# Attention with decay and two expert layers: the state added in PSUM, shared low parts moved to the first expert, alpha loaded ahead, zero matmuls out

## The reference

```python
for t in range(S):                      # attention: B=4, H=8, S=768, D=48
    state = alpha[:, :, t, :, None] * state + einsum('bhd,bhe->bhde', k[:, :, t], v[:, :, t])
    y[:, :, t] = einsum('bhd,bhde->bhe', q[:, :, t], state)
x = y as [3072, 384]
logits = x @ w_gate                     # greedy routing: 8 experts, 384 tokens each
h = relu(x[mask] @ w1[e]);  x[mask] = h @ w2[e]
g = x @ gate2                           # shared by all tokens
out = (g * sigmoid(g) * (x @ val2)) @ out2
```

## Time and profile before

| what | value |
|---|---|
| median of 3 runs | 927.67 us (926.37 to 929.67) |
| the profiled execution | 926.6 us |
| its span | 924.8 us |
| TensorE busy over the span | 854.6 us (92%) |
| VectorE | 528.2 us (57%) |
| ScalarE | 281.0 us (30%) |
| GpSimd | 233.5 us (25%) |
| mean granted TensorE clock | 0.959 of full |

### The profile page before, as it was taken

One profiled execution on the slowest core, in us unless ns is written; L12 is line 12 of the kernel. 1 busy time (PEld: TensorE's weight loads), 2 busy tenths in 40 slices (PEclk: granted clock), 3 DMA queues, 4 the chain that ended last, 5 costly groups with the idle time before them and its releaser, 6 DMA issues.

```text
span 924.8 us, 17511 instructions
## 1 busy us (share of the span) xinstructions
PE 854.6 (92%) x6606; PEld 800.6 (87%) x6606; DVE 528.2 (57%) x1098; ACT 281.0 (30%) x505; POOL 233.5 (25%) x171
## 2 busy tenths in 40 slices
PE   6899998249999999999999999999999999999991
PEld 3778776139999999999999999999999999999990
DVE  7999996654654465446445644563466446543330
ACT  1333333032234323432242224333233332333220
POOL 2433223013051314312340324041405030522001
PEclk7999999559999999999999999999999999999996
DMA  9688863040230023002200320041003002300000
GB/s 342 229 300 302 295 254 111 4 160 1 69 95 23 3 68 94 26 0 85 77 26 0 102 60 26 0 123 44 20 29 116 34 9 68 94 26 1 1 1 29
DMA packets 25570, 77.27 MB, mean 84 GB/s; under 512 B 3776, under 2 KB 10432, under 8 KB 22464
## 3 DMA queue, kind: packets, MB, share of 16 engines
q1 hardware_dynamic: 22464, 67.39, 21.2%
q0 software_dynamic: 3072, 9.44, 3.1%
HBM read 67.38 MB, written 9.44 MB: 83 GB/s over the span
## 4 chain that ended last, share of the span: by engine, by line
PE 76%; DVE 2%; issue 1%; DMA 1%; POOL 0%; ACT 0%; POOLq 0%; ACTq 0%
PE ps_up L1490 45%; PE ps_acc L1490 27%; PE ps_turn L774 2%; DMA x_tok<-x_rows,from_rows 1%; PE ps_turn L794 1%; PE ps_turn L1496 0%; DVE quick_marks_space L699 0%; PE ps_turn L779 0%; DVE quick_marks_space L751 0%; POOL out L1338 0%; PE ps_up L1496 0%; PE ps_acc L1496 0%; POOL x_tok L1310 0%; DVE quick_cut L698 0%; DVE quick_base L693 0%
## 5 line engine op out<-in xcount | busy, mean ns | idle before, releaser
L1316 POOL TENSOR_TENSOR w_low<-w_raw,w_high 128x768 fp32r<-128x768 f32 x60 | 134.8, 2254 | 293.7 <-ACT w_high L1380 293.4
L1490 PE MATMUL ps_up<-z_high,gated_high 128*128 128x384 f32 x576 | 198.1, 344 | 0.2 <-DVE z_low L1447 0.2
L1490 PE MATMUL ps_up<-z_high,gated_low 128*128 128x384 f32 x576 | 193.6, 336 | 0.0
L1490 PE MATMUL ps_up<-z_low,gated_high 128*128 128x384 f32 x576 | 193.4, 336 | 0.0
L1490 PEld LDWEIGHTS ps_up<-z_high,gated_high 128*128 128x128 f32 x576 | 108.2, 188 | 0.9 <-ACT z_high L1393 0.5
L1490 PEld LDWEIGHTS ps_up<-z_high,gated_low 128*128 128x128 f32 x576 | 108.3, 188 | 0.0
L1490 PEld LDWEIGHTS ps_up<-z_low,gated_high 128*128 128x128 f32 x576 | 108.1, 188 | 0.0
L1452 DVE TENSOR_TENSOR act_out<-ps_up,act_out 128x384 f32<-128x384 f32 x96 | 53.6, 558 | 94.4 <-ACT act_out L1396 86.0
L1399 ACT CAST u_high<-act_out 128x384 fp32r<-128x384 f32 x96 | 49.4, 514 | 160.4 <-DVE act_out L1456 160.4
L1490 PE MATMUL ps_acc<-gated_high,u_high 128*128 128x384 f32 x288 | 97.6, 339 | 0.3 <-DVE u_low L1459 0.3
L1490 PE MATMUL ps_acc<-gated_low,u_high 128*128 128x384 f32 x288 | 97.2, 337 | 0.0
(11 more groups left out here) (164 smaller groups left out, 1439.0 us busy)
## 6 DMA issues: line engine op xcount, KB each, us to landing
qka_in<-in_qka SPq DMA_DIRECT2D x24, 1026.0 KB, 7.5
w_raw<-in_experts SPq DMA_DIRECT2D x64, 384.0 KB, 3.1
v_in<-in_v SPq DMA_DIRECT2D x24, 192.0 KB, 7.4
x_rows<-y_rows SPq DMA_DIRECT2D x24, 192.0 KB, 3.6
quick_marks_space<-in_gated SPq DMA_DIRECT2D x6, 576.0 KB, 5.1
gated_raw<-in_gated SPq DMA_DIRECT2D x6, 576.0 KB, 6.1
x_tok<-x_rows,from_rows POOLq DMA_INDIRECT x24
out<-o_tok,to_rows POOLq DMA_INDIRECT x24
```

Source lines behind the costliest of these rows:

```text
L1316: pool.tensor_tensor(w.low[:, m % RING, :], w.raw[:, m % RING, :], w.high[:, m % RING, :].bitcast(F32), ALU.subtract).then_inc(w_low_ready, 1)
L1490: mm = pe.matmul(acc, lhs[a], rhs[b], start=(first and i == 0), stop=(last and i == 2))
```

## The change

It does five things.

1. The state is added in PSUM: for chunks after the first, `update` starts with one matmul of the identity with the state (128 x 192), and the key-value products accumulate on it. `advance` is one instruction that reads PSUM.
2. The two zero matmuls in front of each unit's scores go (the 22 warm-up matmuls at the start stay).
3. All 12 raw chunks of the shared weights have a place of their own during the attention. Only the high parts are cast there.
4. The 12 low parts are made in place by GpSimd in the first expert, between `split_rest(0)` and the splits for expert 1. TensorE waits for each in `gate_and_value`.
5. The first unit's load is cut in three (alpha, reverse alpha, queries and keys), each with a semaphore. The second unit's load comes next, before the identity, the turner, the mask and the first values.

```diff
-            for b in range(B):
-                if b < BUFFERS:
-                    load(b)
+            for cols, landed in ((slice(ALPHA_AT, BACK_AT), alpha0_in), (slice(BACK_AT, QKA), back0_in),
+                                 (slice(0, ALPHA_AT), qk0_in)):
+                sp.dma_start(qka_in[0][:, cols], qka[0, :, cols]).then_inc(landed, 16)
+            load(1)
+            sp.dma_start(idt[:], ident).then_inc(consts_in, 16)
+            sp.dma_start(turner[:], turn_gate).then_inc(consts_in, 16)
+            sp.dma_start(mask[:], causal).then_inc(mask_in, 16)
+            load_v(0, 0)
+            load(2)
+            for b in range(1, B):
                 load_v(b, b)
...
-                    sp.wait_ge(w.gated_low_ready[r], i + 1)
-                    w.load_gated(sp, gated_raw, i + 1, r)
+                    sp.wait_ge(w.gated_high_ready[r], i + 1)
+                    w.load_gated(sp, i + 1, r)
...
-                dve.tensor_tensor(state[b][:, :, :].rearrange("p a e -> p (a e)"), ps_state[:, 0:PAIRS * D],
-                                  state[b][:, :, :].rearrange("p a e -> p (a e)"), ALU.add).then_inc(state_added, 1)
-                dve.wait_ge(state_added, u + 1)
                 end = decay[b][:, :, P:SEG].broadcast_to([P, PAIRS, D])
-                dve.scalar_tensor_tensor(out=state[b][:], in0=state[b][:], scalar=1.0 / DECAY_UNIT, in1=end,
+                dve.scalar_tensor_tensor(out=state[b][:], in0=ps_state[:, 0:PAIRS * D].rearrange("p (a e) -> p a e", a=PAIRS),
+                                         scalar=1.0 / DECAY_UNIT, in1=end,
                                          op0=ALU.mult, op1=ALU.mult).then_inc(state_ready, 1)
...
-                if u % B == 2:
-                    w.split_gated_low(dve, gated_raw, u // B, 0)
...
-                if u % B == 2 and u > B:
-                    w.split_gated_low(pool, gated_raw, u // B - 1, 1)
-            w.split_gated_low(pool, gated_raw, CH - 1, 1)
...
-                    for n in range(FILLERS):
-                        pe.matmul(ps_scores[j % 2][0][:, :], warm[:, 0, 0:P], warm, start=True, stop=True)
...
+                if not first_chunk:
+                    pe.matmul(ps_state[:, 0:PAIRS * D], idt[:, :], state[b][:, :, :].rearrange("p a e -> p (a e)"),
+                              start=True, stop=False)
...
-                                       start=True, stop=True)
+                                       start=(first_chunk and a == 0), stop=(a == PAIRS - 1))
...
+            def expert(e, split_gated=False):
                 split_rest(e)
+                if split_gated:
+                    for j in range(GC):
+                        w.split_gated_low(pool, j // 2, j % 2)
...
             def gate_and_value(e, j):
+                pe.wait_ge(w.gated_low_ready, j + 1)
```

More of the change, by code:

```diff
@@ L87, in attention @@
         qka_loaded = [sem(f"qka_loaded{r}") for r in range(BUFFERS)]
+        alpha0_in = sem("alpha0_in")
+        back0_in = sem("back0_in")
+        qk0_in = sem("qk0_in")
         v_loaded = [sem(f"v_loaded{b}") for b in range(B)]
@@ L315, in step @@
                 if j % B in split_after:
[L316 removed]
+                    w.split_gated_high(act, i, split_after[j % B])
             k_copy(0, 0)
@@ L375, in outputs, with update @@
                 mm.then_inc(y_cols_ready, 1)
-            def update(i, j):
+            def update(i, j, first_chunk):
                 u, b, c = unit(i, j)
                 pe.wait_ge(k_tok_ready, u + 1)
+                if not first_chunk:
+                    pe.matmul(ps_state[:, 0:PAIRS * D], idt[:, :], state[b][:, :, :].rearrange("p a e -> p (a e)"),
+                              start=True, stop=False)
                 for a in range(PAIRS):
@@ L403, in step @@
                         pe.wait_ge(state_ready, u)
-                    update(i, j)
+                    update(i, j, first_chunk)
                 if not first:
@@ L1157, in __init__ @@
         self.gated_high = sb("gated_high", [P, GC, 3 * DM], F32R)
-        self.gated_low = sb("gated_low", [P, GC, 3 * DM], F32R)
         self.gated_in = [sem(f"gated_in{r}") for r in range(2)]
         self.gated_high_ready = [sem(f"gated_high_ready{r}") for r in range(2)]
-        self.gated_low_ready = [sem(f"gated_low_ready{r}") for r in range(2)]
+        self.gated_low_ready = sem("gated_low_ready")
     def add_ring(self, nc, ctx):
@@ L1168, in add_ring, with add_gated_low, load_gated, split_gated_high @@
         self.raw = ctx.enter_context(nc.sbuf_tensor("w_raw", [P, RING, 2 * DM], F32))
-    def load_gated(self, sp, raws, i, r):
-        sp.dma_start(raws[r], self.gated[2 * i + r]).then_inc(self.gated_in[r], 16)
-    def split_gated_high(self, act, raws, i, r):
+    def add_gated_low(self, nc, ctx):
+        self.gated_low = ctx.enter_context(nc.sbuf_tensor("gated_low", [P, GC, 3 * DM], F32R))
+    def load_gated(self, sp, i, r):
+        sp.dma_start(self.chunk(self.gated_raw, i, r), self.gated[2 * i + r]).then_inc(self.gated_in[r], 16)
+    def split_gated_high(self, act, i, r):
         act.wait_ge(self.gated_in[r], 16 * (i + 1))
-        act.copy(self.chunk(self.gated_high, i, r), raws[r]).then_inc(self.gated_high_ready[r], 1)
-    def split_gated_low(self, eng, raws, i, r):
+        act.copy(self.chunk(self.gated_high, i, r),
+                 self.chunk(self.gated_raw, i, r)).then_inc(self.gated_high_ready[r], 1)
+    def split_gated_low(self, eng, i, r):
         eng.wait_ge(self.gated_high_ready[r], i + 1)
-        eng.tensor_tensor(self.chunk(self.gated_low, i, r), raws[r], self.chunk(self.gated_high, i, r).bitcast(F32),
-                          ALU.subtract).then_inc(self.gated_low_ready[r], 1)
+        eng.tensor_tensor(self.chunk(self.gated_low, i, r), self.chunk(self.gated_raw, i, r),
+                          self.chunk(self.gated_high, i, r).bitcast(F32),
+                          ALU.subtract).then_inc(self.gated_low_ready, 1)
     @staticmethod
@@ L1354, in _ @@
                 gather(0, 1)
-                with pool.Fori(0, E - 1) as e:
+                expert(0, split_gated=not again)
+                with pool.Fori(1, E - 1) as e:
                     expert(e)
@@ L1594, in build @@
         quick = QuickRouting(nc, ctx, logits, slot_token, order, failed)
-        attention(nc, qka, v, turn_gate, ident, causal,
-                  x_rows.rearrange("(b c p) n -> b c p n", b=B, p=P), logits, w, quick, consts)
+        with ExitStack() as early:
+            w.gated_raw = early.enter_context(nc.sbuf_tensor("gated_raw", [P, GC, 3 * DM], F32))
+            attention(nc, qka, v, turn_gate, ident, causal,
+                      x_rows.rearrange("(b c p) n -> b c p n", b=B, p=P), logits, w, quick, consts)
+        w.add_gated_low(nc, ctx)
         w.add_ring(nc, ctx)
```

21 lines of the change are left out of this document (11 added, 10 removed).

## The result

The changed kernel takes 935.25 us (median of 7 executions, 931.82 to 939.2), the kernel before 927.69 beside it: ratio 1.0082, 95% interval 1.0067 to 1.0098. It is slower by 0.8%, where 923.0 was predicted. The profiled execution took 938.08 us (span 936.3), 11.5 us above that of before, so it is one of the longer ones of the seven. Ratios and medians leave out one slow execution, of experiment 5, which took 1,686.6 us.

The account below looks back on a forecast made before the run. TensorE was taken to bound an undisturbed unit (5.80 us), VectorE a round of four (24.6 against 23.2). Profiled 926.6 - 13.7 (attention) + 9.0 (expert 0) = 921.9; median 1.07 above, so 923.0, range 913.5 to 929.5.

Parts of the forecast that it names:

- the fourth: Rival, attention: TensorE's unit stays near 5.8 us, identity 0.6, other waits appear, gain only 8 us; 929 us, chance 0.07.
- the third: Rival, attention: without zero matmuls the clock may fall to 1.2 GHz; 935 us for four such units, chance 0.12.
- The expert term: Expert 0: GpSimd's 12 low parts and two-operand VectorE instructions exclude each other, losing 9.0 us.
- the walk: Expert 0, holds followed with old times: L699 stalls 2.0 us, u_low of chunk 0 1.5, of chunk 2 about 5.4.
- Rival 1: Expert 0: the splits cost nothing, as VectorE slips in first or slack takes it all; 914 us, chance 0.17.
- the unit of 5.57 us: Attention, TensorE: a unit goes from 5.80 us, less 0.63 for zero matmuls, plus 0.40 for the identity, to 5.57.
- The identity was taken at 0.40: Attention, TensorE: the 192-column fp32 identity matmul adds 0.40 us a unit, 0.36 at least, 0.60 at the far end.
- The zero matmuls: Attention, TensorE: removing them saves 0.63 us a unit, all of it on the path.
- The stalls: Attention, outputs of unit 4 to 21: 7.0 us of the 105.0 are stalls, and none remain after the change.
- The tail "stays as it is": Attention behind unit 21: it waits for the last shared weights to land and does not change.
- Before unit 4: Attention start: VectorE leads; three units lose 0.39 us and one 1.35 us L1180 goes, 2.5 us; alpha ahead adds 0.5.
- "No per-expert cost": Experts: the 12 added TensorE waits of an expert stand behind long matmuls and cost nothing.

Follow-up runs that it names:

- experiment 5: Kernel before with only the low parts' array allocated behind the small routing arrays, no instruction different: 930.24 us, ratio 1.0037.
- experiment 3: Changed kernel with the last pair of shared weights issued one unit earlier: 931.66 us, ratio 1.0046 to the kernel before.
- experiment 9: Changed kernel with state addition back on VectorE and zero matmuls back, leaving the low parts' move and loads ahead: 932.69 us, ratio 1.0064 to the kernel before.
- experiment 1: Changed kernel with the state added on VectorE again and no identity matmul: 925.17 us, ratio 0.9979 to the kernel before.
- experiment 2: Changed kernel with the two zero matmuls back in front of each unit's scores: 941.43 us, ratio 1.0148 to the kernel before.
- experiment 4: Changed kernel with each low part made in three pieces of 384 columns on GpSimd: 929.28 us, ratio 1.0033 to the kernel before.
- experiment 8: Kernel before with only the identity matmul in and the state addition on VectorE out: 930.77 us, ratio 1.0036.
- experiment 6: Kernel before with only the new order of first loads and the first unit's load cut in three: 926.88 us, ratio 1.0000.
- experiment 10: Changed kernel, addition on VectorE, last shared loads earlier, low parts in pieces, four chunks' made ahead, waits in first expert only: 916.79 us, ratio 0.9894 to kernel before.
- experiment 11: The kernel of experiment 10 plus an unused array of 3,296 bytes a partition ahead of the low parts: 912.29 us, ratio 0.9843 to the kernel before.

## Why the prediction was wrong

It was 923.0, range 913.5 to 929.5; the time is 935.25. Of the rivals, the fourth comes nearest (a unit that stays near 5.8 because the identity takes 0.6, named at 929), and a fall of the clock like the third's came at one place. That the third was named at 935 and 935.25 was measured is chance: it stood for four units at a low clock in the body of the attention, and there are none (1.00 at 48 to 52 and at 80 to 120 us). Point by point:

- **The expert term was right**, its size in part by luck. 9.0 us forecast, 9.3 measured, and two of its three places (L706, the old L699, 4.0 us; u_low 2.4) are among TensorE's waits; the third is the wait for the counts (L790, 1.9), at the end of the chain of two-operand instructions that the walk named. Rival 1 is out. The Trainium skill's page "SBUF — State Buffer", section "Who interferes with whom", lists tensor_scalar among the instructions that can take the shared pair, which my walk left out: the trace agrees with the page (L705 1.06 us in expert 0, L710 2.42, where their medians are 0.24). The sizes inside the sum were off: L706 cost 4.0 us for the 2.0 of the walk, the u_low of chunk 0 1.0 for 1.5, and the counts and the u_low of chunk 2 together 3.3 for 5.4. And the sum hangs on where the parts happen to fall: the same twelve parts cost 9.0 us in the trace of experiment 3, 9.1 in that of 9, 10.8 in 1 and 11.2 in 2. Experiment 4 shows the mechanism: with pieces a third as long the hold of L706 goes from 2.40 to 0.77 us and the loss from 9.3 to 4.9.
- **The failed step is the unit of 5.57 us.** It is the sum of two sizes, both off to the same side. The identity was taken at 0.40; it is 0.52 (experiment 8 alone: 0.53). The zero matmuls were taken at 0.63, and the unit became shorter by only 0.43 without them (experiment 2: 0.43). Together 17 x 0.32 = 5.4 us, the whole of the difference in that stretch (99.5 against 94.1). Both sizes hang on one wrong reading. The load of the first zero matmul (107.56) was taken for the end of the turn's products and the start of the zero matmuls. But that load overlaps the turn's last products, which run until 106.69 + 1.14 = 107.83. The trace of before had the answer. At the end of the attention the turn has no zero matmuls behind it:

```profile
153.42 1.14 PE L390 MATMUL ps_y_rows<-turner,y_cols 128*128 128x104 f32 x8
154.49 1.08 PE L367 MATMUL ps_y_cols<-scores,v_in 128*48 128x128 f32 x16
```

From the turn to the next work it takes 1.07 us there, and 1.50 with the zero matmuls in between, so that these cost 0.43. One of the turn's four products takes 0.27 us, not 0.218, and 192 columns in proportion 0.49. With these two sizes the unit comes to 5.80 - 0.43 + 0.49 = 5.86 us, near the measured 5.89 and above the 5.80 of before. The range of the identity (0.36 to 0.60) held its value, that of the zero matmuls was not bounded at all. This step alone takes the forecast from 923.0 to 928.4, where nothing is gained any more; the tail, the place of the arrays and the gain that did not come before unit 4 lifted the time out of the range.

- **The stalls.** All 7.0 us of them are gone, as forecast (experiment 9: unit 5.80 throughout). But what removed them is the move of the low parts alone (the loads ahead gave nothing, experiment 6). VectorE, relieved of those, takes 4 x 5.18 = 20.7 us a round against TensorE's 23.2; the 0.39 us of the addition didn't need to go anywhere. The prediction costed the edits as one sum and did not ask what each gave when the others were in. In that order they give: low parts moved and loads ahead +5.3 us (experiment 9), zero matmuls out -7.5 (experiment 1), identity in +10.1 (the changed kernel; 8.9 of it in the units, see experiment 1). The sum is +7.9; the comparison of the two kernels gave +7.6.
- **The tail "stays as it is" was wrong**, by 6.0 us in the profiled execution. Relative to the outputs of unit 21 the cast of the last shared pair comes 1.8 us later than before (5.12 against 3.35), and TensorE waits 2.56 us for the copy behind it, where it waited 0.37. Behind this wait the clock falls. Experiment 3 takes away the wait, and the low clock goes too. Whether the zero matmuls would have held the clock is not shown. Experiment 1 has none and keeps 1.00 after a wait of 1.23 us; experiment 2 has them and keeps it after 1.38; and with them the clock fell after 2.42 us in the kernel before and after 2.89 in experiment 5. After the first 30 us a long wait went before each fall in the attention, with the zero matmuls and without, so the rival's reason, the missing zero matmuls, is not needed. Why the pair comes later is not shown either.
- **Before unit 4** 1.6 us came and not 3.0. The fourth unit's scan stood at 21.56, as forecast, with a wait of 1.93 for the forecast 2.5; alpha ahead gave nothing (experiment 6), its forecast was 0.5. VectorE then comes to the mask of unit 4 2.3 us earlier (37.27 for 39.56), near the 2.5 forecast for it. But it does not lead here, as the prediction had it: TensorE works without a wait, and its units take 4.21 us where they took 4.64, which is again the 0.43 of the zero matmuls. The clock at the start adds chance: between 24 and 28 us it was 0.50 here and 0.67 before, and 1.00 in experiment 4, whose attention is that of the changed kernel and whose unit 4 comes at 39.14.
- **"No per-expert cost" was wrong** by 2.2 us over six experts and 0.6 in the last. The waits cost nothing, as forecast (experiment 10 has them out and the same 88.78). The place of the low parts in SBUF does (experiments 5 and 11), which nothing in the diff's instructions tells. Why this distance matters stays open: experiment 11 kept the old distance to the high parts modulo 16 KB, but this fits other rules as well, and no other distance was tried.

The forecast's terms with the measured sizes: 926.6 - 5.5 - 1.6 + 6.0 + 0.4 + 9.3 + 2.9 = 938.1, the profiled execution. The median lies 2.8 below that. It may be that the clock at the tail does not fall in every execution: the two shortest, 931.8 and 931.9 us, have a mean granted clock of 0.962, the other five 0.950 to 0.956. But only one execution has a trace.

## What to carry to other kernels

When two engines are nearly full, find which single item makes the second one the bound, move that, and leave everything else where it is: here TensorE was the tighter one, and 0.52 us put on it to save 0.39 on VectorE cost 10 us, 8.9 of them in the units. Time an instruction by the distance between the same two neighbours with and without it, not from the load of its weights, and look for such a pair at the ends of the stage too. Work for GpSimd beside VectorE goes in short pieces and, if it can, where VectorE is idle (9.3 us lost became 1.9); after every gain, look at which transfer at the stage's end was only just in time, and issue it earlier.

## What the runs showed of the hardware

- The place of an array changes the pace of matmuls with no wait in between: 36 products of 128x384 took 6.44 or 6.54 us with the same instructions, 0.3% of the kernel.
- After the first 30 us of the attention the granted clock fell behind long waits of TensorE, with zero matmuls and without: with them after 2.42 us (0.68 over four us) and 2.89 us (0.57 over eight), without them after 2.56 us (0.50) and 2.89 us (0.58 over eight). After 1.38 us with them and 1.23 us without it stayed at 1.00. They cost 0.43 us a unit, and where TensorE has no wait they do nothing: 1.00 with and without. At the low clock outputs took 1.95 us and not 1.08.
- A VectorE instruction with both operands in SBUF, and a TENSOR_SCALAR as well, stood until GpSimd's instruction ended: L706 3.33 us for 0.93, L710 2.42 for 0.24. With GpSimd's work in pieces of 1.02 us the longest hold of L706 was 0.77 us. Reductions (L696, 0.15 us) were not held.
- One fp32 identity product of 192 columns holds TensorE 0.52 us, in two instructions; four of 104 columns take 1.07 us.
